# Mixture-of-experts pipeline on one core: the first expert's token pick as a TensorE loop over four staged tiles

## The chip, the cores and the metric

The kernel runs on one core of a Trainium2 chip. The metric is the device time of one execution in microseconds (us), the median of 3 runs. One more execution is recorded by the hardware profiler.

## The reference

Three stages, all in float32. First an attention over 4 batches, 8 heads and 576 positions with head size 64; half of the heads look at a local window, the others at every 32nd position. Its output is laid out as 2304 tokens of 512 values. Then a mixture of 8 experts, where a token whose skip score isn't positive is passed on as it is. Last, a feed-forward layer 512 to 2048 to 512 with a piecewise quadratic between. The change touches only the beginning of the second stage:

```python
def _moe_ref(x, w_skip, w_gate, w1, w2):
    do_compute = x @ w_skip > 0
    xc = x[do_compute]
    logits = xc @ w_gate
    e_idx = np.argmax(logits, axis=1)
    probs = softmax(logits)
    gate_w = probs[np.arange(len(xc)), e_idx]
    for e in range(8):
        mask = e_idx == e
        h = np.maximum(xc[mask] @ w1[e], 0.0)
        y[mask] = gate_w[mask, None] * (h @ w2[e])
    out[do_compute] = xc + y
```

## The kernel before, in words

The five engines run instruction streams written by hand, with semaphores between them. Of the sizes, `P` = 128 partitions, `NT` = 18 tiles of 128 tokens, `DC` = 4 chunks of the 512 values of a token, `WIN` = 168 tokens in the window of one expert, `E` = 8 experts.

**Attention** fills `XT`, the tokens with their 512 values along the partitions. TensorE then turns it tile by tile into rows (`rows(t)`, L967), ScalarE copies each of the 18 tiles from PSUM into `xrow` (L572, semaphore `rows_copied`), and VectorE meanwhile computes the logits' maximum, the gates and, for each token, its place in an order sorted by expert (L706 to L733).

**Sorting.** GpSimd scatters the 18 tiles of `xrow` into the DRAM tensor `x_sorted` by 18 indirect DMAs of one tile each (L469, semaphore `scattered`). When all have landed, SyncE reads the second expert's window back (`xsecond`, L380 and L381). When the pick described below is over (`first_picked`), it reads all tokens back in sorted order into `xrow` by 6 DMAs of three tiles (L385, semaphores `sorted_in`). The queue then goes on to w2 of the second expert (L370), the list of further windows (L389), w1 of the third expert (L367), the gates (L396) and the loads of the later experts.

**The pick.** To spare the first expert the way through DRAM, TensorE gathers its tokens by itself. VectorE writes for each tile `t` a table `hot(t)` of 128 by 168 ones and zeros (L736, `hot_ready`), which says for each token whether it goes to slot 0 to 167 of the sorted order. The tables lie in the columns of `XT` that the rows no longer need. TensorE multiplies the rows of a tile with its table and adds up over the 18 tiles in PSUM: the result is the first expert's window, 512 values by 168 tokens, in the four banks `first_b` (L995). The loops are written out in full:

```python
for c in range(DC):
    for t in range(NT):
        if c == 0:
            pe.wait_ge(rows_copied, t + 1)
            pe.wait_ge(hot_ready, t + 1)
        last = pe.matmul(first_b[c][:, 0:WIN], xrow[:, t, P * c:P * (c + 1)], hot(t), start=(t == 0), stop=(t == NT - 1))
    last.then_inc(first_picked, 1)
```

Chunk by chunk, that is 72 products; each float32 product stands as two matmul records and two weight loads in the trace, so 144 and 144. VectorE copies the banks 0 and 2 into `xw` (L765), ScalarE the banks 1 and 3 (L580), each as soon as `first_picked` has counted its chunk, and after VectorE has signalled `more_ready` at the end of its routing work in the case of ScalarE.

**The experts.** `into(0)` on TensorE (L1031) multiplies the window with w1 of the first expert; it waits for all four copies. Then come `second_rows` (L1002, needs `second_in`), `sort_turned` (L1014, transposes of the 18 sorted tiles, needs `sorted_in` piece by piece), `into(1)`, `outof(0)` (L1041) and so on through the experts, and the feed-forward layer (L1077 and L1096). Its groups of 512 tokens run in a loop of three rounds, as do attention's batches; these are the two loops with a branch that TensorE has run through more than once (a third, for windows past the first of an expert, depends on the data).

Of the kernel before, what the change touches and what calls it, by code (L numbers as in the profile page):

```python
# [9 lines left out]
F32 = mybir.dt.float32  # L10
# [8 lines left out]
P = 128  # L19
# [3 lines left out]
D, E, FE, FF = H * HD, 8, 1024, 2048  # L23
N = B * S
NT = N // P
DC, FEC, FFC = D // P, FE // P, FF // P
# [58 lines left out]
WIN = 168  # L85
# [28 lines left out]
def program(nc, qT, kT, vl, vs, wg, w1, w2, win, wout, cst, out):  # L114
    with ExitStack() as ctx:
        def sem(name):
            return ctx.enter_context(nc.semaphore(name))
# [4 lines left out]
        def at(name, shape, dt, offset=None):  # L122
            size = int(np.prod(shape[1:])) * (2 if dt == BF16 else 4)
            size = (size + 63) // 64 * 64
            where = top[0] if offset is None else offset
            t = nc.alloc_sbuf_tensor_at(name, list(shape), dt, offset=where)
            if offset is None:
                top[0] += size
            return t, where, where + size


        XT, _, _ = at("XT", [P, DC, XCOLS], F32)

        WE1, w_at, w_end = at("WE1", [P, 2, DC, FE], F32)
        WE2, _, w_end = at("WE2", [P, 2, FEC, D], F32)
        o = w_at
        q_loc, _, o = at("q_loc", [P, 2, S], F32, o)
        k_loc, _, o = at("k_loc", [P, 2, S], F32, o)
        v_loc, _, o = at("v_loc", [P, LOC, 4 * HD], F32, o)
        q_str, _, o = at("q_str", [P, 2, S], F32, o)  # L140
        k_str, _, o = at("k_str", [P, 2, S], F32, o)
        v_str, _, o = at("v_str", [P, STRIP_PAIRS - 1, 4 * HD], F32, o)
        v_rest, _, o = at("v_rest", [P, 3, 4 * HD], F32, o)
        assert o <= w_end
        WOH, _, o = at("WOH", [P, FFC, D], F32R, w_at)
        WOL, _, o = at("WOL", [P, FFC, D], F32R, o)
        assert o <= w_end

        WIH, r_at, _ = at("WIH", [P, DC, FF], F32R)
        WIL, _, r_end = at("WIL", [P, DC, FF], F32R)  # L150
        xrow, _, o = at("xrow", [P, NT, ROW], F32, r_at)
        prob, p_at, o = at("prob", [P, SLOTS, 512], F32, o)
        probT, _, o = at("probT", [P, 3, 512], F32, o)
        assert o <= r_end
        gateT, _, o = at("gateT", [GATES * E, NT // GATES, P], F32, p_at)
        gates, _, o = at("gates", [P, NT // GATES, GATES * E], F32, o)
        assert o <= r_end

        hid, h_at, _ = at("hid", [P, 2, FEC, WIN], F32)
        xw, _, _ = at("xw", [P, BUFS, DC, WIN], F32)  # L160
        gb, _, _ = at("gb", [P, 2, WIN], F32)
        ytmp, _, h_end = at("ytmp", [P, 2, WIN], F32)
        h_end = top[0] = max(h_end, h_at + 4 * (2 * DC * G + 2 * G))
        raw_in, i_at, i_end = at("raw_in", [P, 2, DC, P], F32)
        raw_out, _, raw_end = at("raw_out", [P, 2, D], F32)

        xsecond, _, o = at("xsecond", [P, 2, D], F32, i_at)
        assert o <= raw_end
        yl, _, o = at("yl", [P, DC, G], F32R, h_at)
        gh, _, o = at("gh", [P, 2, G], F32R, o)  # L170
        yh, _, o = at("yh", [P, DC, G], F32R, o)
        assert o <= h_end
        gl, _, o = at("gl", [P, 2, G], F32R, i_at)
        assert o <= i_end
        cl, _, _ = at("cl", [P, G], F32)
        gr, _, _ = at("gr", [P, G], F32)

        con, _, c_end = at("con", [P, C_END], F32)
        ident = con[:, C_ID:C_ID + P]
        before = con[:, C_UP:C_UP + P]  # L180
        ident_b, _, _ = at("ident_b", [P, P], BF16)
        warm, _, _ = at("warm", [P, 512], BF16, h_at)
        mask_b, _, _ = at("mask_b", [P, MASKS, KEYS], BF16)
        wgs, _, _ = at("wgs", [P, DC, LGW], F32)
        sm, _, _ = at("sm", [P, SLOTS, 32], F32)
        half, _, _ = at("half", [P, 1], F32)
        tok, _, _ = at("tok", [P, NT], U32)
        starts, _, _ = at("starts", [1, E + 1], I32)
        more, _, _ = at("more", [1, 2, EXTRA], I32)
        listed, _, _ = at("listed", [EXTRA, 2], I32)  # L190
        n_more, _, _ = at("n_more", [1, 1], I32)
        pairs, _, _ = at("pairs", [EXTRA, C_SLOT - C_END], F32)
        slot_of, _, _ = at("slot_of", [P, NT], U32)
# [3 lines left out]
        o = h_at  # L197
        lgT, _, o = at("lgT", [P, EARLY + LATE], F32, o)
        lg, _, o = at("lg", [P, NT, E + 1], F32, o)
        top8, _, o = at("top8", [P, NT], F32, o)  # L200
        dif, _, o = at("dif", [P, NT, E], F32, o)
        ex, _, o = at("ex", [P, NT, E], F32, o)
        pick, _, o = at("pick", [P, NT, E], F32, o)
        vmx, _, o = at("vmx", [P, NT], F32, o)
        active, _, o = at("active", [P, NT], F32, o)
        oh, _, o = at("oh", [P, NT, E + 1], F32, o)
        gate, _, o = at("gate", [P, 3, NT], F32, o)
        ones, _, o = at("ones", [P, NE9], F32, o)
        tot, _, o = at("tot", [P, E + 1, NT], F32, o)
        run, _, o = at("run", [P, E + 1, NT], F32, o)  # L210
        base, _, o = at("base", [P, E + 1, NT], F32, o)
        pos3, _, o = at("pos3", [P, NT, E + 1], F32, o)
        posf, _, o = at("posf", [P, NT], F32, o)
        count, _, o = at("count", [EXTRA, E], F32, o)
        has, _, o = at("has", [EXTRA, 2, E, EXTRA], F32, o)
        upto, _, o = at("upto", [EXTRA, E, EXTRA], F32, o)
        begin, _, o = at("begin", [EXTRA, E, EXTRA], F32, o)
        found, _, o = at("found", [EXTRA, 3, E, EXTRA], F32, o)
        value, _, o = at("value", [EXTRA, 2], F32, o)
        slots, _, o = at("slots", [P, WIN], F32, o)  # L220
# [14 lines left out]
        first_b, second_b, sort_b = bank[4:8], bank[2:4], bank[2:6]  # L235
# [17 lines left out]
        rows_ready, rows_copied, logits_ready = sem("rows_ready"), sem("rows_copied"), sem("logits_ready")  # L253
        lgT_ready, lgT_main, lgT_rest = sem("lgT_ready"), sem("lgT_main"), sem("lgT_rest")
        route, dif_ready, oh_ready, exp_ready, ranks_ready, slots_ready, aux_ready, starts_ready = sem("route"), sem("dif_ready"), sem("oh_ready"), sem("exp_ready"), sem("ranks_ready"), sem("slots_ready"), sem("aux_ready"), sem("starts_ready")
        scattered, pads_out = sem("scattered"), sem("pads_out")
        gates_flat = sem("gates_flat")
        slots_in, hot_ready, first_picked, first_copied = sem("slots_in"), sem("hot_ready"), sem("first_picked"), sem("first_copied")
        second_in, second_turned, second_copied = sem("second_in"), sem("second_turned"), sem("second_copied")
        sorted_in = [sem(f"sorted_in{g}") for g in range(NS)]  # L260
# [23 lines left out]
        def hot(t):  # L284

            return XT[:, t % DC, WIN * (t // DC):WIN * (t // DC + 1)]
# [5 lines left out]
        def behind(eng, signal, value):  # L292

            if not (isinstance(value, int) and value <= 0):
                eng.wait_ge(signal, value)
# [5 lines left out]
        def _(sp):  # L301
# [78 lines left out]
            sp.dma_start(xsecond[:, 0, :], xs[bass.ds(start_1, P), 0:D]).then_inc(second_in, 16)  # L380
            sp.dma_start(xsecond[0:WIN - P, 1, :], xs[bass.ds(start_1 + P, WIN - P), 0:D]).then_inc(second_in, 16)  # L381

            sp.wait_ge(first_picked, DC)
            for g in range(NS):
                sp.dma_start(xrow[:, ST * g:ST * (g + 1), :], xs[SORTED * g:SORTED * (g + 1)].rearrange("(t p) c -> p t c", p=P)).then_inc(sorted_in[g], 16)  # L385
            load_w2(1, 1)
# [146 lines left out]
        def _(act):  # L533
# [36 lines left out]
            for t in range(NT):  # L570
                act.wait_ge(rows_ready, t + 1)
                act.copy(xrow[:, t, 0:D], row_b[t % 4][:, :]).then_inc(rows_copied, 1)  # L572
                if t == EXP_AT:
                    act.wait_ge(dif_ready, 1)
                    act.activation(ex[:, :, :], dif[:, :, :], ACT.Exp).then_inc(exp_ready, 1)

            act.wait_ge(more_ready, 1)
            for c in range(1, DC, 2):
                act.wait_ge(first_picked, c + 1)
                act.copy(xw[:, 0, c, :], first_b[c][:, 0:WIN]).then_inc(first_copied, 1)  # L580

            def relus(e, par):
# [69 lines left out]
        def _(dve):  # L652
# [107 lines left out]
            dve.sem_inc(more_ready, 1)  # L760


            for c in range(0, DC, 2):
                dve.wait_ge(first_picked, c + 1)
                dve.tensor_copy(xw[:, 0, c, :], first_b[c][:, 0:WIN]).then_inc(first_copied, 1)  # L765
            dve.wait_ge(second_turned, 1)
            dve.tensor_copy(xw[:, 1, :, 0:P], second_b[0][:, :].rearrange("p (c n) -> p c n", c=DC)).then_inc(second_copied, 1)
# [2 lines left out]
            for t in range(NT):  # L770
                if t % GATES == GATES - ST:
                    dve.wait_ge(sorted_in[t // ST], 16)
                    first = t - GATES + ST
# [77 lines left out]
        def _(pe):  # L851
# [120 lines left out]
            for k, (at_, width, turned_b, signal) in enumerate(((0, EARLY, logit_b, lgT_main), (EARLY, LATE, gate_b, lgT_rest))):  # L972
                pe.wait_ge(signal, 1)
                for q in range(width // P):
                    last = pe.transpose(turned_b[:, STRIPS * LGW * q:STRIPS * LGW * (q + 1)], lgT[0:STRIPS * LGW, at_ + P * q:at_ + P * (q + 1)], ident[0:STRIPS * LGW, 0:STRIPS * LGW])
# [11 lines left out]

            for c in range(DC):  # L990
                for t in range(NT):
                    if c == 0:
                        pe.wait_ge(rows_copied, t + 1)
                        pe.wait_ge(hot_ready, t + 1)
                    last = pe.matmul(first_b[c][:, 0:WIN], xrow[:, t, P * c:P * (c + 1)], hot(t), start=(t == 0), stop=(t == NT - 1))  # L995
                last.then_inc(first_picked, 1)

            def second_rows():
                pe.wait_ge(second_in, 32)
# [191 lines left out]
```

## Time and profile before

| | us |
|---|---|
| median of 3 runs | 687.55 (687.15 to 689.2) |
| the profiled execution, its own time | 690.49 |
| its span in the trace | 688.4 |
| TensorE busy with matmuls | 655.7 (95% of the span) |
| VectorE, ScalarE, GpSimd busy | 317.6, 187.8, 126.1 |
| TensorE in the chain that ended last | 90% of the span |

The profile page lists groups of instructions by source line and engine; the trace answers narrower questions about a stretch of the span. Times in the trace count from the beginning of the span. "PEclk" is the granted clock of TensorE as a share of full speed. A releaser is what ended an engine's idle time; "issue" means that the trace shows nothing the engine was waiting for, and "remote" that no instruction of the trace right before it explains the end of the wait.

### The profile page before, as it was taken

What the parts mean: (1) busy time and instruction counts of PE and PEld (TensorE: products, weight loads), DVE (VectorE), ACT (ScalarE), POOL (GpSimd) and SP (SyncE); (2) the same over time, 40 slices, a digit from 0 to 9 for tenths busy, and PEclk for the clock granted to TensorE, in tenths of its full rate; (3) what the DMA queues carried; (4) which work ended last, traced back from release to release, by engine and by line L of the source; (5) the groups of instructions that cost most, each with busy time, mean ns of one, the idle gap of its engine ahead of it and who ended that gap; (6) DMA issues with size and microseconds to landing.
All of it is one profiled execution on the core that took longest, in us unless ns stands there. A gap on an engine that the chain in (4) does not pass through costs nothing.

```text
span 688.4 us, 12667 instructions
## 1 busy us (share of the span) xinstructions
PE 655.7 (95%) x5265; PEld 567.6 (82%) x5266; DVE 317.6 (46%) x588; ACT 187.8 (27%) x361; POOL 126.1 (18%) x134
## 2 busy tenths in 40 slices
PE   7888995999999999999999999999999999999995
PEld 3776694999999999878888888888888888888994
DVE  4767460042121121676456544456444565545652
ACT  2455440141111111132224222232222332223331
POOL 1333155003222224882000200002000020000201
PEclk9999995999999999999999999999999999999999
DMA  8686595495777775230000100001000010000100
GB/s 279 207 282 206 181 388 186 172 357 160 259 256 261 263 274 189 85 115 17 0 1 1 61 1 0 1 0 61 0 0 0 0 61 0 0 0 1 62 0 31
DMA packets 39469, 76.09 MB, mean 111 GB/s; under 512 B 2967, under 2 KB 18012, under 8 KB 38916
## 3 DMA queue, kind: packets, MB, share of 16 engines
q1 hardware_dynamic: 36548, 66.00, 28.1%
q0 software_dynamic: 2880, 9.52, 3.6%
q8 instruction: 29, 0.48, 0.3%
q14 instruction: 12, 0.10, 0.0%
HBM read 65.57 MB, written 9.94 MB: 110 GB/s over the span
## 4 chain that ended last, share of the span: by engine, by line
PE 90%; DMA 4%; DVE 2%; issue 2%; SPq 1%; POOL 1%; ACT 0%; DVEq 0%
PE pair L1077 28%; PE pair L1096 16%; PE bank L1096 13%; PE pair L1031 11%; PE out_pair L1041 5%; PE bank L1041 5%; DMA k_loc<-kT 2%; PE pair L995 2%; PE out_pair L920 2%; PE pair L878 2%; PE out_pair L995 2%; DMA k_str<-kT 1%; PE bank L898 1%; PE bank L1014 1%; DVE yl L812 1%
## 5 line engine op out<-in xcount | busy, mean ns | idle before, releaser
L1077 PE MATMUL pair<-yh,WIH 128*128 128x512 f32 (+1 forms) x316 | 114.2, 368 | 0.2 <-ACT yh L609 0.2
L1077 PE MATMUL pair<-yh,WIL 128*128 128x512 f32 (+1 forms) x316 | 114.1, 368 | 0.0
L633 ACT ACTIVATE cl<-cl,half 128x512 f32<-128x512 f32 (+1 forms) x80 | 54.4, 680 | 185.1 <-DVE cl L833 183.7
L841 DVE TENSOR_TENSOR gl<-gr,gh 128x512 fp32r<-128x512 f32 (+1 forms) x80 | 54.5, 681 | 73.2 <-ACT gh L642 72.0
L833 DVE TENSOR_SCALAR cl<-pair 128x512 f32<-128x512 f32 (+1 forms) x79 | 50.3, 636 | 71.0 <-PE pair L1077 70.9
L528 POOL DMA_INDIRECT out<-XT,tok x18 | 18.6, 1031 | 349.4 <-DVE XT L821 345.4
L1077 PE MATMUL pair<-yl,WIH 128*128 128x512 f32 (+1 forms) x316 | 77.8, 368 | 0.4 <-DVE yl L812 0.4
L1031 PE MATMUL pair<-xw,WE 128*128 128x168 f32 x512 | 74.3, 306 | 0.5 <-ACT xw L580 0.5
L1031 PEld LDWEIGHTS pair<-xw,WE 128*128 128x128 f32 x512 | 73.3, 190 | 0.7 <-issue 0.7
L642 ACT CAST gh<-gr 128x512 fp32r<-128x512 f32 (+1 forms) x80 | 46.3, 579 | 85.6 <-PE bank L1096 58.3
L1077 PEld LDWEIGHTS pair<-yh,WIH 128*128 128x128 f32 x316 | 59.5, 188 | 11.0 <-ACT yh L609 0.6
L1077 PEld LDWEIGHTS pair<-yh,WIL 128*128 128x128 f32 x316 | 59.5, 188 | 10.3
L1077 PEld LDWEIGHTS pair<-yl,WIH 128*128 128x128 f32 x316 | 56.0, 189 | 10.6 <-DVE yl L812 0.8
L1096 PE MATMUL pair<-WOH,gh 128*128 128x512 f32 x160 | 62.6, 391 | 1.0 <-DVE gl L841 0.9
L839 DVE TENSOR_TENSOR gr<-gr,cl 128x512 f32<-128x512 f32 (+1 forms) x80 | 53.1, 664 | 21.9 <-ACT cl L633 21.6
L1096 PE MATMUL pair<-WOL,gh 128*128 128x512 f32 x160 | 62.4, 390 | 0.0
L1096 PE MATMUL pair<-WOH,gl 128*128 128x512 f32 x160 | 62.1, 389 | 0.0
L1096 PE MATMUL bank<-WOH,gh 128*128 128x512 f32 x128 | 49.8, 389 | 0.0
L1096 PE MATMUL bank<-WOL,gh 128*128 128x512 f32 x128 | 49.8, 389 | 0.0
L1096 PE MATMUL bank<-WOH,gl 128*128 128x512 f32 x128 | 49.8, 389 | 0.0
L836 DVE TENSOR_SCALAR gr<-pair 128x512 f32<-128x512 f32 (+1 forms) x79 | 49.5, 627 | 0.0
L588 ACT ACTIVATE hid<-pair 128x168 f32<-128x168 f32 x64 | 19.9, 311 | 108.3 <-PE pair L1031 108.3
(154 smaller groups left out, 849.6 us busy)
## 6 DMA issues: line engine op xcount, KB each, us to landing
WE<-w SPq DMA_DIRECT2D x16, 2048.0 KB, 10.9
xrow<-x_sorted SPq DMA_DIRECT2D x6, 781.5 KB, 9.8
v_loc<-vl SPq DMA_DIRECT2D x4, 1024.0 KB, 6.7
raw_in<-win SPq DMA_DIRECT2D x16, 256.0 KB, 9.2
raw_out<-wout SPq DMA_DIRECT2D x16, 256.0 KB, 2.6
q_loc<-qT SPq DMA_DIRECT2D x4, 576.0 KB, 5.3
k_loc<-kT SPq DMA_DIRECT2D x4, 576.0 KB, 6.9
v_str<-vs SPq DMA_DIRECT2D x8, 256.0 KB, 4.4
```

The lines of the kernel that those rows point to most:

```text
L588: act.activation(hid[:, par, f, :], hid_b[f % 2][:, 0:WIN], ACT.Relu).then_inc(h_done, 1)
L633: act.activation(cl[:, 0:n], cl[:, 0:n], ACT.Square, bias=half[:, :], scale=0.5).then_inc(squared, 1)
L642: act.copy(gh[:, f % 2, 0:n], gr[:, 0:n]).then_inc(g_high, 1)
L833: dve.tensor_scalar(cl[:, 0:n], h2_of(g, f)[:, 0:n], -1.0, 1.0, ALU.max, ALU.min).then_inc(clamped, 1)
L836: dve.tensor_scalar(gr[:, 0:n], h2_of(g, f)[:, 0:n], 1.0, -1.0, ALU.max, ALU.add).then_inc(over, 1)
L839: dve.tensor_tensor(gr[:, 0:n], gr[:, 0:n], cl[:, 0:n], ALU.add).then_inc(g_ready, 1)
L841: dve.tensor_tensor(gl[:, f % 2, 0:n], gr[:, 0:n], gh[:, f % 2, 0:n].bitcast(F32), ALU.subtract).then_inc(g_low, 1)
L995: last = pe.matmul(first_b[c][:, 0:WIN], xrow[:, t, P * c:P * (c + 1)], hot(t), start=(t == 0), stop=(t == NT - 1))
L1031: last = pe.matmul(hid_b[f % 2][:, 0:WIN], WE1[:, par, c, P * f:P * (f + 1)], xw[:, buf, c, :], start=(c == 0), stop=(c == DC - 1))
L1041: last = pe.matmul(y_b[c][:, 0:WIN], WE2[:, par, f, P * c:P * (c + 1)], hid[:, par, f, :], start=(f == 0), stop=(f == FEC - 1))
L1077: last = pe.matmul(h2_of(g, f)[:, 0:tokens], w[:, c, P * f:P * (f + 1)], x[:, c, 0:tokens], start=(not low and c == 0 and k == 0), stop=(l ...
L1096: last = pe.matmul(fin_b[t][:, :], x[:, f % 2, P * t:P * (t + 1)], w[:, f, :], start=(f == 0 and k == 0), stop=(f == FFC - 1 and k == 2))
```

## The change

TensorE goes tile by tile rather than chunk by chunk, and all but the first and the last tile are done in a loop of four rounds of four tiles. Since a loop body has to name fixed places, ScalarE copies tiles 1 to 16 of `xrow` into a ring of four places, `stage` (8 KB per partition, in room left free by attention). The tables are read where they were, at an address that is computed from the loop's register. TensorE signals each finished tile (`tile_picked`) and ScalarE may fill a place again when the tile that was in it four tiles before is picked. `first_picked` is counted once, at the very end; the four copies into `xw` and SyncE's read-back wait for that.

```diff
@@ memory
+        stage, _, o = at("stage", [P, DC, D], F32, o)
@@ SyncE
-            sp.wait_ge(first_picked, DC)
+            sp.wait_ge(first_picked, 1)
             for g in range(NS):
                 sp.dma_start(xrow[:, ST * g:ST * (g + 1), :], ...).then_inc(sorted_in[g], 16)
@@ ScalarE
+            for t in range(1, NT - 1):
+                behind(act, tile_picked, t - DC)
+                act.wait_ge(rows_copied, t + 1)
+                act.copy(stage[:, t % DC, :], xrow[:, t, 0:D]).then_inc(staged, 1)
+
             act.wait_ge(more_ready, 1)
+            act.wait_ge(first_picked, 1)
             for c in range(1, DC, 2):
-                act.wait_ge(first_picked, c + 1)
                 act.copy(xw[:, 0, c, :], first_b[c][:, 0:WIN]).then_inc(first_copied, 1)
@@ VectorE
+            dve.wait_ge(first_picked, 1)
             for c in range(0, DC, 2):
-                dve.wait_ge(first_picked, c + 1)
                 dve.tensor_copy(xw[:, 0, c, :], first_b[c][:, 0:WIN]).then_inc(first_copied, 1)
@@ TensorE
-            for c in range(DC):
-                for t in range(NT):
-                    if c == 0:
-                        pe.wait_ge(rows_copied, t + 1)
-                        pe.wait_ge(hot_ready, t + 1)
-                    last = pe.matmul(first_b[c][:, 0:WIN], xrow[:, t, P * c:P * (c + 1)], hot(t), start=(t == 0), stop=(t == NT - 1))
-                last.then_inc(first_picked, 1)
+            def pick(rows_of_tile, table, first, last):
+                for c in range(DC):
+                    picked = pe.matmul(first_b[c][:, 0:WIN], rows_of_tile[:, P * c:P * (c + 1)], table, start=first, stop=last)
+                return picked
+
+            pe.wait_ge(rows_copied, 1)
+            pe.wait_ge(hot_ready, 1)
+            pick(xrow[:, 0, :], hot(0), True, False)
+            assert (NT - 2) % DC == 0
+            with pe.Fori(0, (NT - 2) // DC) as i:
+                for t in range(1, DC + 1):
+                    pe.wait_ge(staged, DC * i + t)
+                    pe.wait_ge(hot_ready, DC * i + t + 1)
+                    pick(stage[:, t % DC, :], XT[:, t % DC, bass.ds(WIN * i + WIN * (t // DC), WIN)], False, False).then_inc(tile_picked, 1)
+            pe.wait_ge(rows_copied, NT)
+            pe.wait_ge(hot_ready, NT)
+            pick(xrow[:, NT - 1, :], hot(NT - 1), False, True).then_inc(first_picked, 1)
```

## Rows read from the trace of the kernel before

**Rows 1.** The profile page: TensorE's share and its granted clock in 40 slices

```profile
PE 655.7 (95%) x5265; PEld 567.6 (82%) x5266; DVE 317.6 (46%) x588; ACT 187.8 (27%) x361; POOL 126.1 (18%) x134
...
PEclk9999995999999999999999999999999999999999
```

**Rows 2.** Chain of waits, 91 to 140 us: start us, us, what

```profile
92.35 9.23 PE out_pair L995 x63
101.59 0.41 issue
...
108.86 1.67 issue
...
117.62 10.78 PE pair L995 x58
...
128.42 0.31 ACT xw L580
128.73 0.14 issue
128.86 9.36 PE pair L1031 x64
```

**Rows 3.** TensorE alone in four stretches: busy us, records, granted clock, DMA share, GB/s

```profile
92.19:101.28 9.09, 9.09 (x64) 1.00 1.03 396
101.28:117.62 16.34, 8.07 (x26) 0.62 0.58 221
117.62:122.20 4.58, 4.58 (x16) 0.50 0.26 75
122.20:128.40 6.20, 6.18 (x43) 1.00 0.00 0
```

**Rows 4.** Timeline of GpSimd and SyncE, 91 to 130 us

```profile
91.89 1.14 POOL L469 DMA_INDIRECT x_sorted<-xrow,slot_of  x1 [17.23 <-ACT xrow L572]
...
113.67 0.96 POOL L469 DMA_INDIRECT x_sorted<-xrow,slot_of  x1 [0.30 <-issue]
...
117.61 0.37 SPq L381 DMA_DIRECT2D xsecond<-x_sorted  x1
128.41 4.70 SPq L385 DMA_DIRECT2D xrow<-x_sorted  x6
```

**Rows 5.** DMA queues in the stretches 98 to 101 and 101 to 117 us: packets, MB, share

```profile
q8 instruction: 1, 0.02, 2.0%
...
q0 software_dynamic: 1126, 3.71, 60.5%
q1 hardware_dynamic: 2, 0.00, 0.0%
```

**Rows 6.** Chain of waits in attention, 34 to 37 us, and the DMA queue there

```profile
35.01 1.82 issue
...
q8 instruction: 1, 0.02, 2.2%
```

**Rows 7.** Timeline of VectorE and ScalarE: the four copies of the picked window

```profile
102.72 0.33 DVE L765 COPY xw<-out_pair 128x168 f32<-128x168 f32 x1 [4.58 <-remote]
123.29 0.33 DVE L765 COPY xw<-pair 128x168 f32<-128x168 f32 x1 [20.23 <-PE pair L995]
...
92.28 1.25 ACT L572 COPY xrow<-pair 128x512 f32<-128x512 f32 x2
117.84 0.30 ACT L580 COPY xw<-out_pair 128x168 f32<-128x168 f32 x1 [24.31 <-remote]
128.42 0.30 ACT L580 COPY xw<-pair 128x168 f32<-128x168 f32 x1 [10.28 <-PE pair L995]
```

**Rows 8.** TensorE's timeline at the middle of the pick, 105 to 107 us

```profile
105.59 0.65 PE L995 MATMUL out_pair<-XT,xrow 128*128 128x168 f32 x1 [0.41 <-issue]
```

**Rows 9.** Register work ahead of an instruction with a computed address, VectorE and ScalarE

```profile
L799 DVEq FUSED_REGOPS  x32: 53/57/77, 159.6 to 284.9; - x32
...
L609 ACTq FUSED_REGOPS  x8: 46/46/46, 452.9 to 540.3; - x8
```

**Rows 10.** TensorE over a back edge of the group loop, and instruction packets 39 to 74 us

```profile
454.00:455.00 1.00, 1.00 (x6) 0.82 (x5) 1.00 (x2) 1.00 (x3) 0.00 (x0) 1.00 0.00 0
...
q8 instruction: 1, 0.02, 0.2%
```

**Rows 11.** What follows the pick: VectorE's tables before it, TensorE and DMA after it

```profile
90.80 4.01 DVE L736 TENSOR_SCALAR XT<-slots,posf 128x168 f32<-128x168 f32 x18
...
139.44 1.09 PE L1014 MATMUL bank<-con,xrow 128*128 128x128 f32 x8 [0.42 <-DVE xw L767]
...
147.57 2.59 PE L1031 MATMUL pair<-xw,WE 128*128 128x168 f32 x17
...
DMA packets 387, 0.79 MB, mean 394 GB/s; under 512 B 16, under 2 KB 16, under 8 KB 386
```

More of the change, by code:

```diff
@@ L257, in program @@
         gates_flat = sem("gates_flat")
+        staged, tile_picked = sem("staged"), sem("tile_picked")
         slots_in, hot_ready, first_picked, first_copied = sem("slots_in"), sem("hot_ready"), sem("first_picked"), sem("first_copied")
```

## The prediction

> **What bounds the kernel now.** I read the page first: TensorE is busy for 95% of the span, and its granted clock is full in all slices but the seventh, 103 to 120 us, where it is half [rows 1]. The pick lies in that slice. The chain of waits says that TensorE sets the end there too, but not by work: between 101.59 us and 117.62 us it holds pieces called "issue", up to 1.67 us each, in which TensorE waits for nothing the trace knows [rows 2]. The table of stretches gives their price. In the first 9.09 us the pick runs at 9.09 / 64 = 0.142 us a record. At that pace its 144 records take 20.5 us; they take 128.40 - 92.19 = 36.2 us [rows 3]. So 15.8 us are lost. 58 records are left at 117.62 [rows 2], so 86 were done in 25.4 us, where 12.2 would do: 13.2 us lost by stalling. The last 58 take 10.78 instead of 8.2 us, 2.5 us lost, because the clock is at half until 122.20 [rows 3] (1.2 instead of 2.4 GHz, after the stretch in which TensorE had little to do).
>
> What the change is worth depends on what these "issue" pieces are. Two readings fit at first sight. **Reading F:** TensorE waits for its own instructions, and less straight code (the pick shrinks from 72 products written out to 24) cures it. One instruction packet of 16 KB does land at 98 to 101 us [rows 5], just before the stall. **Reading S:** the scatter holds TensorE's issue and its signals up. GpSimd issues its 18 scatters from 91.89 to 114.63 us, and while TensorE stalls, they are all the traffic there is [rows 4, 5].
>
> Three things speak for S. No instruction packet moves between 101 and 117 us; only the scatter's queue does [rows 5]. Where a missing block surely stopped TensorE, in attention, it looks otherwise: one packet, one gap of 1.82 us, then full speed [rows 6]; in the pick some 20 records trickle through 16 us. And the signals are late as well. Chunk 0, 36 records, is done at 92.19 + 36 x 0.142 = 97.3, some 97.5 us with the last one's tail, yet VectorE, idle since it had finished routing, copies it at 102.72: 5.2 us late. Chunk 1 ends at 105.59 + 0.65 = 106.24, and idle ScalarE copies it at 117.84: 11.6 us late, at the very time when TensorE runs again [rows 7, 8]. Code that isn't there would not delay a signal already sent. Against S stands only that the packet and the scatter's first data come within a few us of each other, so the trace can't part them for the beginning of the stall.
>
> **The change part by part**, by reading S, against the profiled execution's 690.49 us; that one is 2.9 us above the median of 687.55, and I carry the difference over.
>
> - Products: 72 before and after, the same shapes, so 144 records at 0.142 us: 0. The tables are ready long before (18 in 4.01 us from 90.80 [rows 11]), and tile by tile TensorE asks for one only every 8 records = 1.14 us: 0.
> - First stage copy: tile 0 is picked from 92.19 to 93.33 us. ScalarE ends its row copies at 92.28 + 1.25 = 93.53 [rows 7]; a stage copy, costed like these at 1.25 / 2 = 0.63 us, is there at 94.16. TensorE waits 0.8 us. Bounds: 0.6 to 1.2 us, by a copy from SBUF being quicker or slower than one from PSUM. From tile 2 on a copy (0.63) is shorter than a tile (1.14): 0. The 16 copies, 10 us, are hidden in ScalarE's idle time until 117.84 [rows 7].
> - The ring: ScalarE may refill a place only when it knows the tile is picked. At 11.6 us of lateness plus a copy that is 4 tiles in about 13 us, or 0.3 a us; in the stall TensorE does 86 - 64 = 22 records, under 3 tiles, in 16 us, or 0.17 a us. The stall is the tighter limit: 0. If the two add up, see the second rival.
> - Loop: two wait values and one address are computed for each tile. The trace has no such work on TensorE; the nearest rows are VectorE's and ScalarE's, 0.057 and 0.046 us [rows 9]. All 48 on the path give 2.7 us. The lower bound is 0, since TensorE's sequencer runs ahead of its array: over a back edge of the group loop the array isn't idle at all [rows 10]. I take 0.3 us, near the row of the loop.
> - The back edges, three taken: 0, by the same row. Most of attention's loop lies between 39 and 74 us, and one instruction packet lands there in all [rows 10]. The Trainium skill ("Runtime: NRT & Kernel Launch", section "Instruction fetch mechanics") says that a taken branch whose target isn't in the buffered blocks stops the engine until the block is fetched; it also says that crossing a block in straight code is mostly hidden. By its first half the sum would be higher by three gaps, the third rival; here the rows side against it.
> - Copies behind the pick: before, only the last chunk's copy stood between pick and experts (0.31 us and 0.14 [rows 2]). Now each engine has two, one after the other: +0.3 us. The early ones were hidden before, and with `first_picked` at the end that cover is gone.
> - SyncE: the read-back waits for the same moment as before. It has 9.36 us of `into(0)` and then the second window's rows as cover; before, the first transposes waited for VectorE's copy and not for the read-back [rows 11]: 0 for a shift of 1 or 2 us.
>
> Sum: 0.8 + 0.3 + 0.3 = +1.4 us, 691.9 for a profiled execution, **689.0 us** as a median. The stall, and the half clock after it, stay. Own range 687.5 to 690.5: no loss of the three at one end, most of the register work exposed at the other.
>
> **The rivals.**
>
> 1. Reading F holds: no instructions are missing in the loop and the pick runs at 0.142 us throughout, at full clock. It ends at 92.19 + 0.8 + 20.5 + 0.3 = 113.8; with 0.75 us for the copies `into(0)` starts at 114.5 rather than 128.86. Does the rest follow? The read-back can't start before the second window's loads at 117.98 [rows 4]; its 4.7 MB at 394 GB/s take 11.9 us, with an estimated start-up of 1.5 us until 131.4 [rows 11]. TensorE wants the last piece at 114.5 + 9.36 + 1.2 + 6.8 = 131.9. So it just holds, and the gain is 14.3 us: 673.2 us. For it: the instruction packet at 98 to 101. Against it: the trickle and the late signals. A weaker form: the products run free but the signals stay late, so that the ring stops TensorE in between, for a gain of 3 to 12 us.
>
> 2. Slower: the ring binds. The place is ScalarE's wait for `tile_picked`, the price is the signal's lateness. Tiles 1 to 4 are picked by about 98.7 us. If their signals take 11.6 us, 5 to 8 run around 110 and 9 to 12 wait until the scatter is over, at 117 to 118. Then 9 tiles, 72 records, are left instead of 58: +2.0 us at full clock, up to +4 with the longer half clock and a last wait: 691.5 us. It decides as soon as a signal takes longer than TensorE needs for the four tiles ahead of it. Behind that wait stand only ScalarE's two window copies, which need the pick anyway.
>
> 3. Slower: each of the three back edges fetches its block anew, at the 1.82 us of the one known gap [rows 6]: +5.5 us, 694.4 with the rest of the sum. Rows 10 speak against it.
>
> **How the numbers follow.** A measurement of this kernel can tell about 0.3% from no change, that is 2.1 us. The forecast has 0.44 (0.34 within 0.3%, 0.10 slower by a little more). Rival 1 has 0.36, 0.28 in full and 0.08 in its weaker form; it is that high since the stall is the largest loss of this stage and reading S rests on lateness, not on a known cause. Rival 2 has 0.15 and rival 3 has 0.05, both slower. That gives 0.36 faster, 0.34 the same, 0.30 slower. Two signs hold most of the chance, so the range must reach rival 1 in full: 673 to 692 us; below it and above it together lie about 1.5 in 10.
>
> **What would show it.** Right: after the change the "issue" pieces still stand between about 101 and 117 us, the clock falls in the same slice, and the pick ends at 129 to 130 us; ScalarE's stage copies from the fifth on come many us after their tile was picked. A first wait of TensorE on ScalarE of about 0.8 us shows the first term, two copies in a row on each engine the last. Wrong: a pick that runs through in some 21 us while the scatter's queue is busy, with `into(0)` near 115 us and the read-back waiting for the scatter rather than for the pick. Rival 2 shows as TensorE's waits on ScalarE's stage copies in mid-scatter, rival 3 as gaps of nearly 2 us with an instruction packet at each round of the loop.

## The result, and the profile after

The changed kernel takes 690.17 us, the median of 17 runs (688.29 to 693.51), beside 687.55 us for the kernel before in the same runs: a ratio of 1.0040, 95% interval 1.0022 to 1.0058. Repeated in a later job it gave 1.0050 (1.0025 to 1.0075), 691.86 beside 688.21 us. So it is slower by 2.6 us, a little more than the 0.3% that can be told from no change. The forecast was +1.4 us.

First the page of the changed kernel: TensorE's share and its clock, as in [rows 1].

```profile
PE 651.4 (95%) x5266; PEld 565.2 (82%) x5266; DVE 316.2 (46%) x588; ACT 197.6 (29%) x377; POOL 127.1 (18%) x134
...
PEclk9999995999999999999999999999999999999998
```

ScalarE has 16 instructions and 10 us more: the stage copies. The clock falls in the same slice. The chain of waits of the changed kernel (start us, us, what) shows what has become of the "issue" pieces of [rows 2]:

```profile
91.11 0.52 ACT stage L583
91.62 0.25 issue
91.87 0.83 PE out_pair L1000 x4
...
98.97 1.30 issue
...
102.28 0.02 ACT stage L583
102.31 6.99 another core or an unknown queue
109.30 0.02 issue
109.32 0.02 ACT stage L583
109.34 5.62 another core or an unknown queue
114.96 0.02 issue
114.98 0.63 ACT stage L583
...
115.83 1.48 PE out_pair L1000 x4
...
127.27 0.58 DVE xw L773 x2
127.86 0.14 issue
127.99 9.36 PE pair L1049 x64
```

Read it from the top. Tile 0 is over at 91.07, and TensorE stands 0.8 us until the first staged tile is there. At 98.97 us the stall begins. What was "issue" before is now, for 12.6 us, "another core or an unknown queue": the chain goes through ScalarE, and ScalarE waits for TensorE's `tile_picked`; nothing in the trace explains why that comes so late. The same in the timeline of ScalarE (start us, us, what, in brackets the idle time before it and what ended it):

```profile
93.31 0.62 ACT L583 COPY stage<-xrow 128x512 f32<-128x512 f32 x1 [0.16 <-PE pair L1000]
95.18 0.62 ACT L583 COPY stage<-xrow 128x512 f32<-128x512 f32 x1 [1.26 <-PE pair L1000]
99.42 0.62 ACT L583 COPY stage<-xrow 128x512 f32<-128x512 f32 x1 [3.62 <-PE pair L1000]
102.28 0.62 ACT L583 COPY stage<-xrow 128x512 f32<-128x512 f32 x1 [2.25 <-PE pair L1000]
109.32 0.62 ACT L583 COPY stage<-xrow 128x512 f32<-128x512 f32 x1 [6.42 <-remote]
114.98 2.18 ACT L583 COPY stage<-xrow 128x512 f32<-128x512 f32 x4 [5.04 <-remote]
```

and in that of TensorE:

```profile
100.27 0.83 PE L1000 MATMUL out_pair<-XT,stage 128*128 x4 [1.30 <-issue]
...
103.13 1.49 PE L1000 MATMUL out_pair<-XT,stage 128*128 x4 [1.46 <-issue]
...
110.19 1.49 PE L1000 MATMUL out_pair<-XT,stage 128*128 x4 [4.45 <-ACT stage L583]
115.83 1.48 PE L1000 MATMUL out_pair<-XT,stage 128*128 x4 [3.04 <-ACT stage L583]
```

Behind the first wait these are all of TensorE's gaps in the pick, 10.3 us in four, and all four are waits for the ring, also the two that the trace calls "issue". At 98.97 us TensorE has picked the tiles 0 to 6, and the copy of tile 7 ends at 99.42 + 0.62 = 100.04; TensorE starts on it 0.23 us later. The next three starts come 0.23, 0.25 and 0.23 us after the end of their copy. The copies in turn come later and later after the tile that they wait for: tile 5 is copied at once when tile 1 is picked, tile 6 0.8 us after tile 2, then 3.9, 5.6 and 11.5 us late, and tile 10 is copied at 114.98, 16.0 us after tile 6 was done at 98.97. So this trace shows late signals from TensorE, but it doesn't show TensorE's own issue trickle.

The whole trace runs 2.4 us ahead of the one before when the pick begins (89.77 against 92.19 us), which has nothing to do with the change; so stages must be compared by their length. From the pick's first record to `into(0)` it is 127.99 - 89.77 = 38.2 us after, and 128.86 - 92.19 = 36.7 before. In a second pair of traces, both from one chip of a later job, it is 128.90 - 89.88 = 39.0 against 125.21 - 89.50 = 35.7. Behind it the chain is the same in both kernels.

One more thing in this trace bears on the two readings. These are all DMA queues of the changed kernel from 91 to 127 us, the whole pick but its first tile:

```profile
q0 software_dynamic: 1440, 4.80, 34.4%
q1 hardware_dynamic: 736, 2.41, 17.3%
q14 instruction: 1, 0.01, 0.1%
```

No packet of q8 moves; that is the queue of 16 KB blocks, of which the kernel before has 29 and the changed one, with fewer TensorE instructions, 28. The loop fetches nothing, and TensorE stalls all the same. Reading F in full, where the pick then runs through, is dead by this. Its weaker form, products that run free but a ring that late signals stop, looks just like this trace, except that nothing is gained; the experiments have to decide on it.

### The profile page after: what moved, and what is told of

Its sections match the earlier page's. It is cut to its first block, busy times and chain, and to the rows that moved or that the text cites. A ratio compares the mean times of both kernels' runs of the same rounds, so it can differ in the third digit from the quotient of the medians.

```text
span 688.0 us, 12725 instructions
## 1 busy us (share of the span) xinstructions
PE 651.4 (95%) x5266; PEld 565.2 (82%) x5266; DVE 316.2 (46%) x588; ACT 197.6 (29%) x377; POOL 127.1 (18%) x134
## 4 chain that ended last, share of the span: by engine, by line
PE 85%; DMA 6%; DVE 3%; another core or an unknown queue 2%; ACT 2%; issue 1%; POOL 1%; SPq 1%; DVEq 0%
PE pair L1095 28%; PE pair L1114 16%; PE bank L1114 13%; PE pair L1049 10%; PE out_pair L1059 5%; PE bank L1059 5%; DMA WE<-w 2%; DMA k_loc<-kT 2%; PE out_pair L928 2%; PE pair L886 2%; PE out_pair L1000 2%; PE pair L1000 1%; ACT xrow L574 1%; DMA k_str<-kT 1%
```

## The experiments

There were 12 runs, four in each of three jobs, each job on a chip of its own. The chips were of two kinds. In the second and third the kernel before took 688.2 and 688.6 us, as in the measurement of the change; in the first it took 678.6 us (675.16 to 685.91, 23 runs), and the two kernels traced there with the scatter beside the pick had no stall. The ratios are within a job throughout.

**The scatter held back.** The kernel before, with one wait more on GpSimd:

```diff
             pool.wait_ge(aux_ready, 2)
+            pool.wait_ge(first_picked, DC)
             for t in range(NT):
                 pool.wait_ge(rows_copied, t + 1)
```

> The kernel before, with one wait more: GpSimd issues the 18 scatters only when the pick is over. Reading S (the scatter holds up TensorE's issue and signals): the pick of 144 records runs through in about 20.5 us at full clock, no issue pieces in it, VectorE's and ScalarE's copies follow their chunk within 0.1 us; into(0) starts some 14 us earlier than 128.86 us, and trickles in its turn once the scatter's data moves. The scatter lands about 25 us after the pick, so the whole kernel is slower by 5 to 12 us. Reading F (missing instructions): the straight-line pick stalls after the same 60 or so of its 144 records, whatever GpSimd does, and takes about 36 us.

It fell on the chip of 678.6 us, with 1.029 (1.024 to 1.034), 19 us slower where 5 to 12 were expected. Its pick takes 20.7 us, but on this chip two other kernels didn't stall beside the scatter either, so that it tells nothing apart. So once more on a chip of 688.6:

> e1_scatter_late once more, since its first run fell on a chip where nothing stalls. On a chip where the kernel before takes about 688 us, reading S says: pick of 20.5 us with no issue piece and with prompt copies, as TensorE's stall goes with the scatter and not with the place in the code; then into(0) beside the scatter trickles, so that it takes 15 to 25 us rather than 9.4. Total 1.02 to 1.04.

1.015 (1.011 to 1.019), less than the 1.02 to 1.04 expected. TensorE in two stretches of this kernel, the pick and `into(0)` (columns as in [rows 3]):

```profile
91.40:112.00 20.60, 20.60 (x146) 1.00 0.29 117
112.50:122.00 9.50, 9.40 (x64) 1.00 0.44 170
```

and the packets of its "instruction" queue from 91 to 112 us:

```profile
q8 instruction: 1, 0.02, 0.3%
```

The same straight code, with a block fetched in the middle of it, runs through at full clock once the scatter isn't there, on a chip where the kernel before and the straight ring below, in the same job, show the slow time. That is reading S, and it rules out the weaker form of reading F too. The second half of the expectation failed: `into(0)`, beside the scatter that GpSimd issues from 113.12 us on, isn't slowed. But the signals are, on ScalarE's timeline of that kernel:

```profile
118.55 0.31 ACT L589 ACTIVATE hid<-pair 128x168 f32<-128x168 f32 x1 [0.83 <-PE pair L1032]
120.20 0.31 ACT L589 ACTIVATE hid<-pair 128x168 f32<-128x168 f32 x1 [1.34 <-PE pair L1032]
123.06 0.31 ACT L589 ACTIVATE hid<-pair 128x168 f32<-128x168 f32 x1 [2.55 <-PE pair L1032]
126.63 0.31 ACT L589 ACTIVATE hid<-pair 128x168 f32<-128x168 f32 x1 [3.26 <-remote]
```

These go with TensorE's f-groups, 1.14 us apart; due at 119.69, 120.83 and 121.97, they come 0.5, 2.2 and 4.7 us late. On the chip of 678.6 us the same eight come 1.14 us apart to the last. In the kernel before, TensorE's first gap comes 9.7 us after the first indirect DMA [rows 2, 4]; here `into(0)` is over 8.9 us after it, and then TensorE has nothing to issue. So signals get late first, and TensorE stops a few us later; in the kernel before, too, chunk 0's signal was due at 97.5 us and hadn't reached VectorE when TensorE's first gap began at 101.59. The Trainium skill ("TensorE: Matmul & The Clock Gate", opening table) gives TensorE a queue of 64 instructions; by an estimate from that figure it would hold 32 records and their weight loads, 4.6 us at the pace of the rows, which fits the order of the two. No run here shows the depth.

**The loop held against a scatter held back.** The same wait in the changed kernel:

> The changed kernel with the scatter held back until the pick is over. Reading S: the loop runs its 144 records in about 21 to 22 us, with one wait of 0.8 us for the first staged tile and no others; ScalarE's stage copies follow tile_picked within 0.1 us; back edges show no gap. If back edges cost a fetch each, three gaps of about 1.8 us show. Total as e1_scatter_late, plus or minus 1 us.

1.038 (1.033 to 1.044), in the first job; worse by 6 us than the other, where 1 was allowed. Both have two runs. Of the 4.8 us between their traces 1.5 stand at the end of the last expert (294.36 against 292.86 us), and the other 3.2 come in the change from the experts to the feed-forward layer, from there to about 310 us, where the edit touches nothing: TensorE waits 2.0 us for VectorE there, where it was 0.8. Why stays open. The pick is as expected: from 90.94 to 112.68 us, 21.7 us. Its waits, from 89 to 114 us (engine, what, who: us in total, times, longest):

```profile
ACT stage L584 <- PE pair L1001: 5.9, 12, 0.5
...
PE out_pair L1001 <- DVE XT L745: 0.8, 1, 0.8
PE pair L1050 <- DVE xw L774: 0.8, 1, 0.8
```

Two waits of TensorE, and no third: beside the 20.7 us of the straight pick and the 0.8 us of the first wait, 0.2 us are left for the loop and its three back edges. The first wait ends when a stage copy is through; that it is put down to VectorE's table is the trace's guess. The twelve waits of ScalarE are the ring breathing, 0.5 us each, under cover.

**The parts of the change.** The ring without the loop: the four rounds written out.

```diff
-            with pe.Fori(0, (NT - 2) // DC) as i:
-                for t in range(1, DC + 1):
-                    pe.wait_ge(staged, DC * i + t)
-                    ...
+            for t in range(1, NT - 1):
+                pe.wait_ge(staged, t)
+                pe.wait_ge(hot_ready, t + 1)
+                pick(stage[:, t % DC, :], hot(t), False, False).then_inc(tile_picked, 1)
```

> The changed kernel with the loop written out: ring of four staged tiles and handshake as they are, 18 tiles in straight code. Reading S: the same picture as the changed kernel, pick of 37 to 38 us, total within 0.2% of it, so 1.002 to 1.006 of before; the loop was worth nothing. Reading F: the stall grows by what the loop had saved. If the loop's register work and back edges were the extra cost, this one is quicker than the changed kernel by up to 1 us.

> The changed kernel without its loop, once more. On a chip of 688 us: ratio 1.002 to 1.008, as the changed kernel had 1.004 and 1.005, and waits of TensorE on ScalarE's stage copies in mid-scatter of some 5 to 10 us in all: the ring's handshake over late signals is the cost, the loop is worth nothing either way. Had the loop helped (fewer instructions to fetch), this one would be slower than 1.008. On a chip of 678 us: 0.998 to 1.001, as before.

On the chip of 678.6 us 0.998 (0.9955 to 1.0006), below what was expected, since nothing stalled there; on that of 688.6 us 1.0016 (0.9992 to 1.0041), just under the 1.002 expected. On the latter the chain has the same two holes as the looped kernel, in straight code:

```profile
101.12 6.29 another core or an unknown queue
...
107.46 7.73 another core or an unknown queue
```

and TensorE's gaps behind its first wait are three, 11.8 us in all where 5 to 10 were expected, each again at the end of a stage copy:

```profile
107.44 0.62 ACT L583 COPY stage<-xrow 128x512 f32<-128x512 f32 x1 [5.71 <-remote]
...
108.11 1.49 PE L1000 MATMUL out_pair<-XT,stage 128*128 128x168 f32 x4 [4.92 <-issue]
```

Here TensorE starts 0.05 us after the copy's end, in all three; in the looped kernel it was 0.23 to 0.25. So the loop's register work does cost something, 0.2 us each time that TensorE stands waiting, and its first wait is 0.59 us in straight code where it is 0.80 in the loop. From the first record to `into(0)` it takes 127.64 - 89.92 = 37.7 us. Whether the loop shows in the whole kernel's time stays open: 1.0016 and the looped 1.0050 come from different jobs and their intervals overlap. That it saves nothing is clear.

The order without the ring: tile by tile from `xrow`, `first_picked` at the end, in straight code.

> The kernel before with the order changed alone: tile by tile in straight code, first_picked once at the end, no stage, no ring. My terms give +0.3 us for the two copies in a row and nothing for the first stage copy: 1.0005 of before. If all of the changed kernel's +0.4% came from the order and the late signal, it shows 1.004 here; if from the ring, about 1.000.

0.9995 (0.9969 to 1.0022), as expected, but on the chip of 678.6 us, where it says nothing of the stall. TensorE from 89.5 to 110.2 us, at full clock:

```profile
89.50:110.20 20.70, 20.66 (x146) 1.00 0.85 318
```

Beside it the scatter runs as ever, and two q8 packets land at 98 to 115 us. So neither the scatter nor a fetch stalls anything on that chip.

**Both kernels once more, traced in one job.**

> The kernel before, unchanged, profiled in this job beside the changed one. In e2_straight_ring and e3_tile_order the scatter ran beside the pick and nothing stalled, at 676 to 678 us, where the kernel before took 678.6 in the same job and not 687.5. So either the 16 us of issue pieces come and go with the chip or the execution (then this trace has none, the pick takes 20.5 us and into(0) starts near 112 us), or they belong to the straight chunk-by-chunk pick (then they are here, and 678.6 is something else).

> The changed kernel, unchanged. Reading S, kept: the stall is a matter of the chip or the execution; where the kernel before has none, this one has none, the loop runs its pick in 21.5 to 22 us, and the ratio is 1.001 to 1.003 for the first stage copy and the two copies in a row (0.8 + 0.3 us). If the loop costs something by itself the ratio here is above e2_straight_ring's 0.998 by more than 0.3%. Reading F: the ratio is 0.98.

The job had the slower kind of chip (688.21 us). The kernel before against itself gave 0.999 (0.9955 to 1.0025), the changed one 1.0050. Both traces show the stall: TensorE is busy for 5.84 of the 14 us from 101 to 115 in the one, for 5.53 in the other. In the changed kernel the four gaps again end 0.22 to 0.25 us after a stage copy. The chain of this trace calls the longest of them, 6.30 us, "issue".

**Bytes or descriptors.** The 18 indirect DMAs kept, but with 36 bytes of a row in place of 2084:

```diff
-                pool.indirect_dma_start(xs, ..., xrow[:, t, :], None).then_inc(scattered, 16)
+                pool.indirect_dma_start(x9, ..., xrow[:, t, AUX:ROW], None).then_inc(scattered, 16)
```

> The kernel before with the same 18 indirect DMAs of 128 rows, but 9 values (36 bytes) of a row rather than 521: the tokens' values aren't scattered nor read back (the read-back is of those 9 values, the second window's rows come from the weights), so the experts compute on unsorted tokens; instruction counts are the same. If the amount of data written disturbs TensorE, no issue pieces and no late signals; if GpSimd's issuing of indirect DMAs and its descriptors do, they stay.

One run of 687.28 us, beside 688.21. TensorE from 101 to 116 us:

```profile
101.00:116.00 15.00, 8.13 (x31) 0.70 0.03 3
```

and the traffic of all queues in that time:

```profile
DMA packets 352, 0.05 MB, mean 3 GB/s; under 512 B 352, under 2 KB 352, under 8 KB 352
```

With the DMA engines at 3% TensorE is still idle for 6.9 of 15 us, and ScalarE still gets chunk 1, done at 101.81 us, only at 116.75. It isn't the bytes. The reverse, the bytes without the indirect DMAs: 18 plain DMAs of the same tiles from SyncE, issued from 94.70 to 106.63 us.

```diff
+            for t in range(NT):
+                sp.wait_ge(rows_copied, t + 1)
+                sp.dma_start(xs[P * t:P * (t + 1)], xrow[:, t, :]).then_inc(scattered, 16)
             sp.wait_ge(scattered, 16 * NT)
```

> The kernel before, but the 18 tiles go to x_sorted by 18 plain DMAs from SyncE's queue, unsorted, and GpSimd issues none: the same 4.8 MB from the same places at the same time; the experts then get tokens in the wrong order. On a chip where the kernel before takes about 688 us: if GpSimd's indirect DMAs (their descriptors, not their bytes) hold TensorE up, the pick runs through in 20.5 us with prompt signals, and the total falls by 8 to 14 us; if any traffic to x_sorted did it, the issue pieces stay. On a chip of the other kind (about 678 us) nothing stalls either way and the run says nothing on it.

0.977 (0.973 to 0.981): 672.86 us beside 688.57, 15.7 us less where 8 to 14 were expected. TensorE in it from 101 to 112 us:

```profile
101.00:112.00 11.00, 10.73 (x76) 1.00 1.04 295
```

and the queue that carries the rows, from 95 to 113 us:

```profile
q1 hardware_dynamic: 2797, 5.60, 99.9%
```

The DMA engines are full, TensorE runs at full clock with no gap, `into(0)` starts at 112.21 us. So on these chips what holds TensorE's instructions and signals up is GpSimd's indirect DMAs, whatever they carry. Whether it is their being indirect, GpSimd's issuing them or the queue they go by (q0 rather than q1) wasn't tried apart.

**Around the stall.** If the pick can't end before 124 to 128 us, the first window may as well come back from DRAM like the second. No tables, no pick; `xfirst` is read at the end of the scatter, transposed and copied, and the read-back of all tokens no longer waits for anything but the scatter.

```diff
-            sp.wait_ge(first_picked, DC)
+            sp.dma_start(xfirst[:, 0, :], xs[0:P, 0:D]).then_inc(first_in, 16)
+            sp.dma_start(xfirst[0:WIN - P, 1, :], xs[P:WIN, 0:D]).then_inc(first_in, 16)
```

> The pick taken out: the first window is read back from x_sorted beside the second one as soon as the scatter has landed, and transposed; the read-back of all tokens follows at once. into(0) can start about 4 us after the scatter's end (116.6 us in the first trace), so near 121 us, with a cold clock for some us. Where the pick stalls until 128 us that gains 4 to 6 us; where the pick runs free and ends near 112 us it loses about 8 us, 1.012.

0.9951 (0.9919 to 0.9984), a gain of 3.7 us where 4 to 6 were expected. `into(0)` starts at 119.91 us, where the pick's kernel in the same job has 125.21. TensorE in it, with the clock as the third number, before `into(0)` and in its first 5 us:

```profile
117.00:121.00 4.00, 2.78 (x12) 0.50 0.94 293
119.91:124.91 5.00, 5.00 (x25) 0.71 1.02 385
```

Then with eight spare products in the gap, to warm the clock:

> e6_through_dram (0.9951 on a chip of 688 us) with 8 spare products of 512 columns between the scatter's end and the arrival of the first window, about 3.4 us at half clock, so that TensorE's clock rises sooner: into(0) takes 9.4 to 10 us rather than 10.8 and the transposes some 1.2 rather than 1.7. Ratio 0.991 to 0.994 on a chip of 688 us; on one of 678 us, where the pick would end by 110 us, 1.005 to 1.01.

0.9911 (0.9876 to 0.9946), the best of the kernels here that leave nothing out, on this kind of chip, and quicker than both the kernel before and the changed one. But not for the reason I gave. In its trace the scatter and all that follows come 3.1 us later, `into(0)` at 123.00; the same two stretches:

```profile
117.00:121.00 4.00, 3.54 (x9) 0.50 0.54 130
123.00:128.00 5.00, 5.00 (x22) 0.62 1.00 368
```

The clock in the first 5 us of `into(0)` is lower after the spare products than it was without them, `into(0)` takes 11.2 us rather than 10.8, and the transposes before it 1.64 rather than 1.70. The intervals of the two kernels overlap, so that the difference isn't shown to be one. On a chip of the other kind neither was run. There, in the trace of the tile order, `into(1)` starts at 132.48 us, and here at 140.03, so that by an estimate from the two this way would lose some 8 us.

## Why the prediction came out as it did

**The bottleneck: right.** The choice of reading S over F carried the forecast, and for the kernel before all three of its grounds hold: no instruction packet during the stall, the trickle, the late signals. The last was the strongest; the lateness follows the scatter to another place in the program. In the changed kernel only the late signals are seen, and the ring turns them into TensorE's waits. I gave reading F 0.36 in all, and it would have cost 17 us. What I hadn't seen is how narrow S is: not the scatter's data, but the indirect DMAs, and only on some chips.

**First stage copy, +0.8 us: right in sum.** 0.80 us in the timeline. But 0.2 us of it are the loop's register work, since the same wait takes 0.59 us in straight code.

**Copies behind the pick, +0.3 us: right.** From the last record to `into(0)` it takes 127.99 - 127.25 = 0.74 us, where it was 128.86 - 128.40 = 0.46.

**Register work and back edges, +0.3 us: near it on a chip without a stall** (0.2 us in the loop with the scatter held back). Beside the scatter it is 0.2 us at each of TensorE's five waits; in the first and the last of them nothing covers it. The back edges cost nothing: no gap, and no packet on q8 at any of the three. The Trainium skill ("Runtime: NRT & Kernel Launch", section "Instruction fetch mechanics") has a taken branch stop the engine for a fetch only where its target isn't in the buffered blocks; this loop, whose body has 64 matmul and weight-load records, fetches nothing and isn't that case, and no run here shows it.

**The ring, 0: the wrong mechanism, and luck with the number.** "The stall is the tighter limit: 0." I took it that TensorE's trickle would hide the ring. There was no trickle to hide it: every gap of TensorE in the pick is a wait for a stage copy. I had priced the ring at 0.3 tiles a us from a lateness of 11.6 us; the lateness grew to 16.0 us, and the ring let three tiles through in the 16.9 us from 98.97 to 115.83. The stalled straight code had done 22 records, under three tiles, in 16. That the two are so nearly equal nothing in my working foresaw; both end when the scatter has landed, as SyncE's next load shows, which goes out at 116.87 us in the kernel before and at 114.25 in the changed one. What is left as a difference is the count at the end. In the changed kernel 80 records are done 26.1 us after the pick's beginning, in the kernel before 86 after 25.4 us [rows 2]; in the second pair it is 80 after 26.2 us against 92 after 25.3. With what the terms of the first copy and the copies behind the pick explain (1.1 us) taken off the lengths above, 0.4 us in the first pair of traces and 2.2 us in the second are left for ring and loop together. The two traces of the kernel before differ by 1.0 us themselves, so no closer figure can be had; nor was the tile order without the ring run on a chip with the stall, which would part the ring from the order there. The median of +2.6 us lies between the two pairs' 1.5 and 3.3. So it is the second rival's mechanism that ran, with 64 records left where it had 72, at 0.4 to 2.2 us where it was priced at +2 to +4.

**The verdict.** 690.17 us lies inside the forecast's own range of 687.5 to 690.5. The likeliest case was "within 0.3%", and the measured +0.4% lies just on the other side; its interval reaches across.

**The look of it.** I expected "issue" pieces to stand as before. What stands under that name are waits for stage copies, and in the first trace most of the time is entered under ScalarE's wait for TensorE. The name that a trace gives to a wait in a ring can change from one execution to the next; the fixed 0.23 us after each copy doesn't.

## What to carry to other kernels

Before curing a stall that the trace can't explain, look at what isn't stalled: here idle engines got signals 5 to 12 us late, and no fetch fell into the gap, which spoke against missing instructions before any run. Where a wait has no cause in the trace, or "issue" for one, line its end up with the ends of the other engines' work: the same short distance every time gives the semaphore away. Don't tie two engines into a tight ring in a stretch where signals are late; a ring is as fast as its depth divided by the lateness, and the lateness can grow, here from 0 to 16 us over six tiles. And where an engine can't use the time it has, ask whether its work is needed there at all: on the chips with the stall, leaving the pick out gained 0.5 to 0.9%, where looping it gained nothing.

## What the runs showed of the hardware

- On some chips GpSimd's indirect DMAs slow down TensorE's issuing (86 records in 25.4 us where 12.2 would do) and its signals to other engines (up to 16.0 us late), even at 36 bytes a row and 3% load on the DMA engines; plain DMAs from SyncE at full load don't. The same kernel takes 688 us there and 678.6 us on a chip where the two kernels traced show nothing of it. What differs between the chips is open.
- Signals get late before TensorE stops: by 0.5, 2.2 and 4.7 us over the last three groups of a stretch of 9.4 us, none of which is itself slower.
- The lateness goes one way: while TensorE's signals reach ScalarE up to 16 us late, ScalarE's reach TensorE in time, 0.05 us after the copy's end in straight code and 0.23 to 0.25 in the loop. Where on the way TensorE's signals are held isn't shown.
- TensorE's clock was at half during the stall. It was back at full from 122.20 us in the kernel before and from 120.0 us in the changed one, where TensorE had run without a gap since 117.62 and 115.83 us. Eight products of 512 bf16 columns in the gap before `into(0)` didn't bring the full clock forward: its mean over the first 5 us of `into(0)` was 0.62 with them and 0.71 without.
